# Attention stage: even units' keys summed ahead of the normalising on GpSimd, values' tails summed by fours

## The reference, cut to what matters

```python
q_d = q.reshape(B, H, Sd, 4, D).mean(axis=3)      # k_d, v_d alike; Sd = 144
out_d = sm_attn(q_d, k_d, v_d)                    # attention over 144 pooled keys
out_up = np.repeat(out_d, 4, axis=2)
mask = np.abs(pos[:, None] - pos[None, :]) < 4    # a band of 7 keys
out_local = softmax(where(mask, scale * q @ k.T, -1e9)) @ v
return out_up + out_local
```

## Time and profile before

| | us |
|---|---|
| median of 3 runs | 689.97 (688.26 to 690.58) |
| profiled execution | 683.98 |
| its span | 682.2 |
| TensorE matmul busy | 664.3 (97%) |
| VectorE busy | 422.3 (62%) |
| ScalarE busy | 325.7 (48%) |
| GpSimd busy | 282.2 (41%) |

### The profile page before, as it was taken

One profiled execution on the slowest core, in us unless ns is written; L12 is line 12 of the kernel. 1 busy time (PEld: TensorE's weight loads), 2 busy tenths in 40 slices (PEclk: granted clock), 3 DMA queues, 4 the chain that ended last, 5 costly groups with the idle time before them and its releaser, 6 DMA issues.

```text
span 682.2 us, 13003 instructions
## 1 busy us (share of the span) xinstructions
PE 664.3 (97%) x5002; PEld 570.3 (84%) x5002; DVE 422.3 (62%) x763; ACT 325.7 (48%) x687; POOL 282.2 (41%) x342
## 2 busy tenths in 40 slices
PE   5999999999999999999999999999999999999998
PEld 4777778888998989999899988888778888888886
DVE  7999859545765566555544322455787556855671
ACT  5999962343454366443442211137365454445432
POOL 6999803020795437554000000586355333542100
PEclk9999999999999999999999999999999999999999
DMA  8989791000000000000200001012100000000001
GB/s 263 255 269 271 184 369 38 0 1 1 1 0 1 1 1 1 1 1 1 62 2 1 1 0 61 1 32 63 31 16 16 31 32 31 1 32 31 32 17 47
DMA packets 26115, 37.54 MB, mean 55 GB/s; under 512 B 2512, under 2 KB 12742, under 8 KB 26054
## 3 DMA queue, kind: packets, MB, share of 16 engines
q1 hardware_dynamic: 26054, 36.71, 17.3%
HBM read 31.98 MB, written 4.72 MB: 54 GB/s over the span
## 4 chain that ended last, share of the span: by engine, by line
PE 91%; DVE 2%; ACT 2%; issue 2%; POOL 2%; DMA 0%; SPq 0%; ACTq 0%; POOLq 0%; DVEq 0%
PE psum L967 29%; PE psum L919 16%; PE psum L1080 14%; PE psum L1057 12%; PE psum L953 12%; PE psum L1066 2%; PE psum L819 1%; PE psum L851 1%; POOL prob L683 1%; PE psum L899 1%; PE psum L838 1%; PE psum L861 1%; PE psum L866 0%; ACT pprob L1141 0%; PE psum L878 0%
## 5 line engine op out<-in xcount | busy, mean ns | idle before, releaser
L967 PE MATMUL psum<-ghi,whi 128*128 128x512 f32 (+1 forms) x320 | 118.2, 370 | 0.0
L967 PE MATMUL psum<-glo,whi 128*128 128x512 f32 (+1 forms) x320 | 118.1, 369 | 0.0
L967 PE MATMUL psum<-ghi,wlo 128*128 128x512 f32 (+1 forms) x320 | 117.7, 368 | 0.0
L1216 ACT ACTIVATE g_sb<-psum 128x512 f32<-128x512 f32 (+1 forms) x48 | 25.3, 527 | 135.5 <-PE psum L919 134.7
L1598 DVE CAST ghi<-g_sb 128x512 fp32r<-128x512 f32 (+1 forms) x48 | 23.5, 490 | 102.2 <-PE psum L967 87.2
L919 PE MATMUL psum<-xhi,whi 128*128 128x512 f32 (+1 forms) x256 | 85.6, 365 | 0.5 <-ACT g_sb L1216 0.3
L1603 DVE TENSOR_TENSOR glo<-g_sb,ghi 128x512 fp32r<-128x512 f32 (+1 forms) x80 | 66.2, 828 | 19.6 <-ACT ghi L1242 18.0
L967 PEld LDWEIGHTS psum<-ghi,wlo 128*128 128x128 f32 x320 | 60.3, 189 | 10.3
L967 PEld LDWEIGHTS psum<-ghi,whi 128*128 128x128 f32 x320 | 60.5, 189 | 9.7 <-issue 0.4
L919 PE MATMUL psum<-xlo,whi 128*128 128x512 f32 (+1 forms) x192 | 68.0, 354 | 0.0
L967 PEld LDWEIGHTS psum<-glo,whi 128*128 128x128 f32 x320 | 60.5, 189 | 8.8
(11 more groups left out here) (175 smaller groups left out, 1607.2 us busy)
## 6 DMA issues: line engine op xcount, KB each, us to landing
wraw<-w_dram SPq DMA_DIRECT2D x12, 512.0 KB, 7.9
qkT<-qT_dram SPq DMA_DIRECT2D x16, 288.0 KB, 3.6
qkT<-kT_dram SPq DMA_DIRECT2D x16, 288.0 KB, 5.0
out_dram<-ob SPq DMA_DIRECT2D x18, 256.0 KB, 2.0
vw<-v_dram SPq DMA_DIRECT2D x15, 280.0 KB
v<-v_dram SPq DMA_DIRECT2D x16, 256.0 KB, 4.7
wraw<-w_dram SPq DMA_DIRECT2D x16, 256.0 KB, 7.1
b<-w_dram SPq DMA_DIRECT2D x4, 512.0 KB, 4.2
```

Source lines behind the costliest of these rows:

```text
L967: ins = nc.tensor.matmul(psum[:, YB + m, 0:size], a[:, w], b[:, (t * F1 + f) % GR, 0:size], start=(f == 0 and n == 0), stop=(f == F1 - 1 a ...
L1216: nc.scalar.activation(g_sb[:, f % HR, 0:size], psum[:, HB1 + f % HB, 0:size], ACT.Mish).then_inc(g_ok, 1)
```

## The change

- GpSimd sums queries and keys in separate pairs of adds. Keys of even units from 4 on come ahead of the normalising of unit u-1 in step u = unit-1; keys of unit 2 come after it, and unit 1's keys, which VectorE summed before, are summed by GpSimd after unit 1's queries.
- The values of unit 0 and the first tails move from step 0 into step 1, behind unit 2's queries; the values of units 1 and 2 both stand in step 2, behind the third unit's queries (unit 3).
- Tails are loaded into 32-row parts and summed for four units at once, in steps 1, 4, 8 and 12. TensorE takes its 32 rows for the tail product, and transposes up to 112 columns for it.
- SyncE issues queries and keys ahead of the values in each step. It loads four tails in step 2, and later two tails in step s where s % 4 is 3, behind a wait for the last tail sum, and two more in the step after it.

```diff
@@ SyncE
             for s in range(UNITS + 3):
+                if s < UNITS:
+                    wait(sp, l_scored, s + 1 - RQ)
+                    wait(sp, p_scored, s + 1 - RQ)
+                    sp.dma_start(qkT[:, s % RQ, 0, 0:SEQ], qT_d[s]).then_inc(ld_qk[s % RQ], 16)
+                    sp.dma_start(qkT[:, s % RQ, 1, 0:SEQ], kT_d[s]).then_inc(ld_qk[s % RQ], 16)
                 if 1 < s < UNITS + 2:
                     u = s - 2
                     wait(sp, pool_v, u - 1)
...
-                    if u == 0:
-                        sp.wait_ge(rest_ok, 2)
-                    if u % 2 == 0:
-                        wait(sp, pool_vt, u // 2)
-                        for h in range(2):
-                            tail = v_d[u + h][POOLF * P:SEQ].rearrange("(p t) c -> p (t c)", t=POOLF)
-                            sp.dma_start(vt4[h * HD:h * HD + PT, :], tail).then_inc(ld_vt4, 16)
-                if s < UNITS:
...
+                if s == 2:
+                    sp.wait_ge(rest_ok, 2)
+                    load_tails(0, FOUR)
                 if s > 2:
                     load_windows(s - 3)
+                if s > 2 and s % FOUR == FOUR - 1 and s + 1 < UNITS:
+                    sp.wait_ge(pool_vt, (s + 1) // FOUR)
+                    load_tails(s + 1, 2)
+                if s > 2 and s % FOUR == 0 and s < UNITS:
+                    load_tails(s + 2, 2)
@@ GpSimd
+            def pool_two_adds(u, a, dst, ok):
+                halves = half_qk[:, a].rearrange("p (i r) -> p i r", r=2)
+                four = qkT[:, u % RQ, a, 0:SEQ].rearrange("p (i r) -> p i r", r=4)
+                own(nc.gpsimd.tensor_tensor(halves, four[:, :, 0:2], four[:, :, 2:4], ALU.add))
+                nc.gpsimd.tensor_tensor(dst[:, u % 2, 0:POOLED], halves[:, :, 0], halves[:, :, 1], ALU.add)\
+                  .then_inc(ok, 1)
...
+            def pool_four_tails(u):
+                four = u // FOUR
+                pool.wait_ge(ld_vt4, 16 * FOUR * (four + 1))
+                wait(pool, pool_vt, four)
                 own(nc.gpsimd.tensor_tensor(half_vt[:], vt4[:, 0:2 * P], vt4[:, 2 * P:4 * P], ALU.add))
-                wait(pool, p_valued, u - 2)
-                nc.gpsimd.tensor_tensor(vdt[:, two % 2, :], half_vt[:, 0:P], half_vt[:, P:2 * P], ALU.add)\
+                wait(pool, p_valued, u - FOUR)
+                nc.gpsimd.tensor_tensor(vdt[:, four % 2, :], half_vt[:, 0:P], half_vt[:, P:2 * P], ALU.add)\
                   .then_inc(pool_vt, 1)
...
             for u in range(UNITS + 1):
+                if u % 2 == 1 and 2 < u + 1 < UNITS:
+                    pool_keys(u + 1)
                 if u > 0:
                     normalise_local(u - 1)
-                if 0 < u + 1 < UNITS:
-                    pool_queries_keys(u + 1)
-                if u < UNITS:
+                if u == 1:
+                    pool_keys(2)
+                if u + 1 < UNITS:
+                    pool_queries(u + 1)
+                if u == 0:
+                    pool_keys(1)
+                elif u == 1:
+                    pool_values(0)
+                    pool_four_tails(0)
+                elif u < UNITS:
+                    if u == 2:
+                        pool_values(1)
                     pool_values(u)
-                    if u % 2 == 0:
-                        pool_two_tails(u)
+                    if u > 0 and u % FOUR == 0:
+                        pool_four_tails(u)
@@ TensorE
-                k0 = P - par * HD
+                k0 = P - u % FOUR * QP
...
-                pe.wait_ge(pool_vt, u // 2 + 1)
-                half = slice(par * HD, (par + 1) * HD)
+                pe.wait_ge(pool_vt, u // FOUR + 1)
+                part = slice(u % FOUR * QP, (u % FOUR + 1) * QP)
@@ VectorE
-                if u < UNITS - 1:
+                if 0 < u < UNITS - 1:
                     if u % 2 == 0:
                         pool_keys(u + 1)
```

More of the change, by code:

```diff
@@ L44 @@
 PT = POOLED - P
+FOUR = 4
+QP = P // FOUR
 QPAD = (NPB - 1) * PB + HD
@@ L558, in load_w_out, with load_tails @@
                 sp.dma_start(wraw[:, IN1 + c * WB:IN1 + (c + 1) * WB], w1_d[2 * KD + c]).then_inc(ld_wo[c], 16)
-            for s in range(UNITS + 3):
+            def load_tails(u, n):
+                for i in range(u, u + n):
+                    at = i % FOUR * QP
+                    tail = v_d[i][POOLF * P:SEQ].rearrange("(p t) c -> p (t c)", t=POOLF)
+                    sp.dma_start(vt4[at:at + PT, :], tail).then_inc(ld_vt4, 16)
+            for s in range(UNITS + 3):
+                if s < UNITS:
[3 more added lines that the diff above has]
+                    sp.dma_start(qkT[:, s % RQ, 1, 0:SEQ], kT_d[s]).then_inc(ld_qk[s % RQ], 16)
                 if 1 < s < UNITS + 2:
@@ L645, in _, with pool_queries @@
             own(nc.gpsimd.memset(mhalf[:], -0.5))
-            def pool_queries_keys(u):
-                par = u % 2
+            def pool_two_adds(u, a, dst, ok):
[4 more added lines that the diff above has]
+                  .then_inc(ok, 1)
+            def pool_queries(u):
                 pool.wait_ge(ld_qk[u % RQ], 32 * (u // RQ + 1))
@@ L651, in pool_queries_keys, with pool_keys @@
                 wait(pool, pool_q, u)
[L652 to L659, removed]
+                pool_two_adds(u, 0, qd, pool_q)
+            def pool_keys(u):
+                pool.wait_ge(ld_qk[u % RQ], 32 * (u // RQ + 1))
+                wait(pool, p_scored, u - 1)
+                wait(pool, pool_k[u % 2], u // 2)
+                if u == 2:
+                    pool.wait_ge(pool_k[1], 1)
+                pool_two_adds(u, 1, kd, pool_k[u % 2])
             def pool_values(u):
@@ L882, in value_pooled @@
                     rows = slice(h * HD, (h + 1) * HD)
-                    ins = nc.tensor.matmul(turned[rows, OD0:OD0 + POOLED], vdt[half, u // 2 % 2, rows],
-                                           pprobT[half, 1, :, h, :], start=False, stop=True)
+                    ins = nc.tensor.matmul(turned[rows, OD0:OD0 + POOLED], vdt[part, u // FOUR % 2, rows],
+                                           pprobT[part, 1, :, h, :], start=False, stop=True)
                 ins.then_inc(p_valued, 1)
```

5 lines of the change are left out of this document (1 added, 4 removed).

## The result

The changed kernel takes 693.5 us (median of 6 runs, 692.52 to 694.72). Six runs of the kernel before, on the same chip and among them the three known already, have a median of 688.3 (684.39 to 690.58). The ratio on record is 1.0107, with a 95% interval of 1.0083 to 1.0132: slower by 0.8 to 1.3%, some 7 us. It is not the quotient of these two medians, which would be 1.0076 (5.2 us). The forecast was 694.4 and slower.

What follows compares the result with a forecast made beforehand. TensorE was taken to wait on GpSimd, busy without gaps; the late start of unit 6's scores (37.55 against 33.48) plus two four-unit periods of 19.46 instead of 19.27 gave +4.4 on 689.97: 694.4 us, range 690.6 to 697.

Steps and rivals of the forecast that it cites:

- What bounds the kernel: Attention stretch, 18 to 85 us: four engines about equally busy, so order of work sets the pace; TensorE waits for GpSimd.
- the shift of S(14): Start of unit 14's pooled scores on TensorE, taken as measure of the end: from 72.02 to 76.47, +4.4 us.
- GpSimd's sum: GpSimd's work: four tail sums go, unit 1's keys and seven separate keys steps come, net -2.0 us, not gained as time.
- The start: First steps on GpSimd: unit 1's keys at 9.55 cost nothing, 0.8 us idle, unit 2's scores 0.27 early, values(0) end 15.03.
- The queue behind the tails: SyncE's step 3 wait for the first tail sum delays unit 2's values to 22.3; GpSimd stalls 2.5 us, normalise(2) 4.55 late.
- Normalise to scores: From GpSimd's start of normalising to TensorE's next even scores, transposes between: 2.6 us, putting unit 4's scores at 27.25.
- Four units: Later steps: saved tails meet a 0.9 us wait for VectorE's reciprocals(7); four units take 19.46 us instead of 19.27.
- The number: Whole kernel: 4.4 us put on the runs' median of 689.97 gives 694.4 us, slower.
- Rival 1: TensorE's wait for keys is all that counts and goes: six pairs give -3.2 us, 686.8 us; chance 9%.
- rival 2: Queue wait does not bite, unit 2's values landed by 19.8: +1.9 us, 691.9 us; chance 13%.
- Rival 3: Stall comes, but GpSimd then runs without a gap, no reciprocal waits: +2.6 us, 692.6; 16% with a sooner landing included.
- rival 4: Loads stay late after the idle DMA gap, or values(6) and (10) miss: 1 to 2 us more, 696; chance 7%.

Runs made afterwards that it cites:

- 4: Kernel before with only the tails loaded into 32-row parts and summed by fours in steps 0, 4, 8 and 12; ratio 1.0009 to the kernel before.
- 1: Changed kernel without the wait in step 3, all four tails loaded a step later behind the other loads; ratio 1.0047 to the kernel before.
- 2: Changed kernel with even units' keys back behind the normalising, the queue's wait left in; ratio 1.0123 to the kernel before.
- 3: Kernel of 1 with the tail sums in steps 1, 5, 9 and 13, ahead of the values; ratio 1.0011 to the kernel before.
- 5: Kernel of 3 with the values' load put back ahead of queries and keys in each step; ratio 1.0027 to the kernel before.
- 7: Kernel before with queries and keys summed apart and even keys from unit 4 on ahead of the normalising; ratio 1.0010 to the kernel before.
- 6: Kernel of 5 with values(0) in step 0, unit 1's keys on VectorE, values(1) and first tails in step 1; ratio 0.9999 to the kernel before.
- 8: Kernel before with only values(0) and the first tails moved to step 1 and values(1) to step 2; ratio 1.0047 to the kernel before.
- 11: Kernel before, unchanged, profiled a second time; that execution took 690.12 us, against a median of 685.1 of 29 runs beside it.
- 10: Kernel of 9 with VectorE's pooled adds behind the denominators and these tokens' splits a step later; ratio 1.0038 to the kernel before.
- 9: Kernel of 4 with the tail sums in steps 1, 5, 9 and 13, ahead of the values; ratio 1.0032 to the kernel before.
- 12: Kernel before with only VectorE's pooled adds behind the denominators and the splits a step later; ratio 1.0008 to the kernel before.

## Why the prediction was right, and where its sizes were off

**What bounds the kernel, and the shift of S(14).** Right: 9.27 us at S(14) and 9.3 in the span. Only the "almost without a gap" behind S(14) holds for some executions and not for others: the first profile of before has a pause of 1.00 us there, and the second one of 3.03.

**GpSimd's sum.** Right: less work, no gain. 4 shows it by itself.

**The start.** Right but for its sizes. Unit 1's keys were done at 9.2 and took 1.17 us in two adds (8.01 to 9.18; 1.12 forecast). An estimate by the factor of about 2 that the Trainium skill gives (GPSIMD Engine Reference, Engine selection) would have made 1.48 of the 0.74 of VectorE's reduction. The trace disagrees with it here; but that factor is for one operation on either engine, and here two adds stand for a reduction. GpSimd then idled 2.19 us, where 0.8 was forecast; 1 us of that is the late first load of this profile, and in 1, 2, 3 and 5, with first loads at 4.29 to 4.50, it was 0.41 to 1.14.

**The queue behind the tails: this is the step that decided, right in kind and too small.** The tails were forecast at 16.35 and the values at 18.1; they went at 17.34 and 19.11, the same spacing, one late first load further on. But the landing was put at 4.2 us after the issue, and it was 5.7, over the upper bound of 5.5 that the earlier trace rows gave. Those rows end at 40 us; of the whole kernel before, the loads of values landed after 3.4 to 7.3. So the stall was 4.02 instead of 2.5, and normalise(2) came at 27.24 instead of 24.65: 1.0 from the first load, 1.5 from the landing. The windows of unit 1 were to land by about 24, and TensorE went on with them at 25.96; this hid under the wait for normalise(2), as forecast. The estimate from the Trainium skill's figures (DMA: Bandwidth & Descriptors, Bandwidth, and Latency and other measured facts), a landing 2.2 us after the issue, lay further off on the same side.

**Normalise to scores.** 2.6 was forecast for normalise(2) to S(4), and 3.69 measured. The 1.1 is the clock at 0.50, a term that the sum lacked. The late scores probably made VectorE late too, and GpSimd waited 0.53 for a buffer and 0.27 for reciprocals(4): normalise(3) to normalise(4) took 7.15 instead of 6.29. Together with 3.08 from there to S(6), which waited 0.28 for a pooled eviction, S(6) stood at 41.48 instead of 37.55: 2.59 + 0.86 + 0.48.

**Four units.** The mechanism was right: GpSimd waits 0.98 us for reciprocals(7), 0.9 forecast, and there are 6.24 us from there to normalise(8) (58.69; forecast 6.29) and 2.58 to S(10) (2.6). Eight units took 39.81, forecast 38.92. Of the 0.89 more, 0.40 is that normalise(7) started 10.97 after S(6), not 10.57, with its reciprocals; why they were late stays open, and normalise(5) had to wait 0.82 as well, which had not been foreseen. And 0.63 lies between normalise(11) and (12) (6.92 for 6.29), where GpSimd waits 0.87 for values(12) at 75.03. That is a term that the sum lacked. The two loads that it did look at, values(6) and (10) behind the tail waits, waited nothing and 0.32, within its "nothing, at most 0.5 each". Values(12) are behind no tail wait, but behind queries and keys(14); they were issued at 68.28 and took 6.7 us to land. That such waits go when the values come first is what 5 against 3 shows.

**The number.** 4.4 was the sum; the profile after has 9.3, 1.0 of which is the first load. What was missing is 1.5 in the landing, 1.3 between normalise(2) and S(6), mostly from the clock, and 0.9 in the eight units. That the clock is behind most of the 1.3 is argued from the order of the rows; no run had the stall without the slow clock. That 694.4 still lies within 1 us of the 693.5 measured is luck: it stands on 689.97, where the median of before was 688.3 in six runs, and the base that was too high made up for a loss that was too small. On 688.3 the same sum gives 692.7. The forecast's ratio of 1.0064 lies below the interval of the measured 1.0107.

**The rivals.** Rival 1 falls with 7 (keys ahead alone: nothing gained) and rival 2 with 4.02 us of stall. Rival 3 had the stall, but the waits for reciprocals that it left out came. The first half of rival 4, loads that stay late, did come: 1.5 us of landing. Of the total loss, 1 puts 0.6% on the wait at the queue. The split of the remaining 0.47% stays open. The start has some 0.3% (6 against 5, and 8 with 0.47% for itself and its waits at the queue), moving the tail sum takes off 0.36% (3 against 1), and putting the values first takes off the waits but no time (1.0027 in 5, 1.0011 in 3). Each of these is about as large as its interval, and they don't add up. Tails by fours and the keys ahead cost and gain nothing that can be measured (4, 7).

## What to carry to other kernels

A single load queue makes every wait in it a wait of everything behind it: before a producer of such a wait is moved later, look at what is queued behind, and ask what its consumer will stand still for. Work taken off an engine is worth what its neighbours let it use; where four engines are equally busy, as here, ask for each wait that goes which result is late next. And a stall that leaves TensorE without work can cost more than its length: here the granted clock fell to 0.50 behind it, and the transposes that ran at it put the next scores 1.1 us later.

## What the runs showed of the hardware

**A load took longer than the bytes ahead of it explain.** Unit 2's values took 5.7 us to land, though little moved before 19.8 us (0 to 150 GB/s from 18 us on). From there to 24.8 the DMA view's slices add up to some 1.4 MB. What was issued up to the values is 0.9 MB (tails, queries, keys, values); the rest is windows, queries and keys issued behind them. That this sharing is the reason for 5.7 instead of 4.2 is argued from these sums, and no run tried it. Of the whole kernel, loads of values land after 4.0 to 7.2 us (median 5.5), where in the kernel before it was 3.4 to 7.3 (median 4.7):

```profile
L579 SPq DMA_DIRECT2D v<-v_dram x16: 328/430/1738, 3.5 to 82.3; - x16
...
DMA to landing us min/median/max: 4.0/5.5/7.2
```

**The clock.** It fell to 0.50 shortly before 27.0 us, after TensorE had been nearly idle from 22.7 on (in 11, at about 79.2, after one pause of 3.03 us), and was back at 1.00 some 6.8 us later in both. In that time five transposes took 1.75 times as long (1.33 for 0.76).

**TensorE's own pauses.** Within a group of matmuls that no wait divides, TensorE stood still for 1.00 us up to 80.52 in the first profile of before, for 3.03 in the second, and at least once, for 0.66 to 4.22, in the profile of every other experiment. The longest are 4.22 in 10, 3.39 in 2, 3.29 in 9, 2.18 in 8 and 1.70 in 12. Within the eight units lie 1.22 in 1, 1.93 together in 3, 0.94 in 4, 1.33 together in 5, 1.80 together in 6 and 1.07 in 7. The profile of after has none over 0.6 up to 90 us. A 16 KB transfer of the instruction queue lies 2.2 to 3.5 us ahead of the end of every one of these pauses, and in the microsecond ahead of that transfer the DMA engines' share was 0.78 to 1.29. As an example, this is part of the DMA view of 11, 76.5 to 78.2 us, with the pause ending at 79.33:

```profile
q1 hardware_dynamic: 188, 0.30, 57.7%
q8 instruction: 1, 0.02, 4.8%
```

From 70 to 76.5 us that queue moved nothing. Such transfers are not always followed by a pause: the profile of after has 12 of them between 18 and 90 us. None lies in that place ahead of the end of its 3.25 us at 25.96, which fits a wait for the windows. TensorE running out of instructions because their load was held up behind data fits all of this, but no run varied the load of the queues alone, so it stays a conjecture. It matters for reading: such pauses differ between executions of one kernel (1.00 and 3.03 us in the two profiles of before, whose times ran from 683.14 to 691.52 us in 29 runs), and an effect below about 0.3% can't be told from them here.
